# Three fp32r products for the hash bits of a bucketed attention, and another place for the chain behind them

## The reference, cut to what matters

```python
# q, k, v: (2, 8, 768, 64); proj: (64, 6)
q_bits = (einsum('bhsd,dk->bhsk', q, proj) > 0)
k_bits = (einsum('bhsd,dk->bhsk', k, proj) > 0)
q_bucket, k_bucket = sum(q_bits * 2**arange(6)), sum(k_bits * 2**arange(6))
mask   = q_bucket[:, :, :, None] == k_bucket[:, :, None, :]
scores = where(mask, q @ k.T / 8, -1e9)
attn   = exp(scores - scores.max(-1));  attn /= attn.sum(-1) + 1e-9
x      = attn @ v                       # 16 heads, 768 tokens each
x = moe(x)                              # 512 -> 2048 -> 512, leaky relu
x = moe2(x)                             # 512 -> 2048 -> 512, rational function
```

## Time and profile before

| | us |
|---|---|
| profiled execution | 849.61 |
| its span, first to last instruction | 847.6 |
| TensorE busy in it | 816.2 |
| VectorE busy | 575.8 |
| ScalarE busy | 426.7 |
| GpSimd busy | 283.7 |
| end of the first head (L571) | 50.30 |
| end of the thirteenth head | 252.47 |
| end of the last head | 293.75 |

### The profile page before, as it was taken

One profiled execution on the slowest core, in us unless ns is written; L12 is line 12 of the kernel. 1 busy time (PEld: TensorE's weight loads), 2 busy tenths in 40 slices (PEclk: granted clock), 3 DMA queues, 4 the chain that ended last, 5 costly groups with the idle time before them and its releaser, 6 DMA issues.

```text
span 847.6 us, 11624 instructions
## 1 busy us (share of the span) xinstructions
PE 816.2 (96%) x3740; PEld 651.6 (77%) x3740; DVE 575.8 (68%) x886; ACT 426.7 (50%) x639; POOL 283.7 (33%) x365
## 2 busy tenths in 40 slices
PE   8899999999999799999999999998999999999996
PEld 5577777877778678888888888886788788887884
DVE  5578778787887455445333544359998788879885
ACT  1577768777777711112011210136676666667663
POOL 5366655636545499600000044555600000000000
PEclk9999999999999999999999999999999999999999
DMA  6465664575555243200000012122100100010001
GB/s 161 122 191 150 153 157 128 149 173 142 143 131 122 70 144 121 78 1 1 0 1 1 1 50 75 54 72 74 50 2 0 50 0 0 0 49 2 0 1 49
DMA packets 33988, 60.77 MB, mean 72 GB/s; under 512 B 10016, under 2 KB 12192, under 8 KB 33952
## 3 DMA queue, kind: packets, MB, share of 16 engines
q1 hardware_dynamic: 33952, 60.30, 25.9%
HBM read 29.51 MB, written 3.19 MB: 39 GB/s over the span
## 4 chain that ended last, share of the span: by engine, by line
PE 55%; DVE 6%; ACT 2%; issue 2%; DMA 1%; DVEq 0%; ACTq 0%
PE ps_h L980 28%; PE acc L998 27%; DVE work L1137 1%; DVE num L1141 1%; DVE num L1125 1%; DMA out<-stage 1%; DVE g_lo L1102 1%; DVE work L1131 1%; ACT work L1055 1%; DVE den_q L1118 1%; ACT work L1052 1%; DVE num L1121 0%; DVE x_lo L1150 0%; ACT g_hi L1032 0%; ACT work L1041 0%
## 5 line engine op out<-in xcount | busy, mean ns | idle before, releaser
L1032 ACT ACTIVATE g_hi<-num 128x512 fp32r<-128x512 f32 x96 | 60.9, 634 | 219.2 <-PE acc L998 200.7
L1108 DVE TENSOR_SCALAR num<-ps_h,alpha_sb 128x512 f32<-128x512 f32 x48 | 36.0, 751 | 135.7 <-PE ps_h L980 135.7
L754 DVE TENSOR_REDUCE row_max<-ps_a 128x1 f32<-128x384 f32 x192 | 97.9, 552 | 23.4 <-PE ps_a L411 22.5
L551 ACT ACTIVATE ps_s<-ps_s 128x768 f32<-128x768 f32 x96 | 76.7, 798 | 52.5 <-PE ps_s L446 52.0
L782 DVE TENSOR_TENSOR p_lo<-ps_s,p_hi 128x768 fp32r<-128x768 f32 x96 | 90.8, 946 | 16.6 <-ACT p_hi L555 16.6
L555 ACT ACTIVATE p_hi<-ps_s 128x768 fp32r<-128x768 f32 x96 | 78.0, 812 | 4.6
L1102 DVE TENSOR_TENSOR g_lo<-num,g_hi 128x512 fp32r<-128x512 f32 x96 | 73.6, 767 | 8.1 <-ACT g_hi L1032 1.4
L980 PE MATMUL ps_h<-x_hi,w_late_in_hi 128*128 128x512 f32 (+1 forms) x288 | 79.0, 396 | 0.0
L980 PE MATMUL ps_h<-x_hi,w_late_in_lo 128*128 128x512 f32 (+1 forms) x288 | 78.8, 396 | 0.0
L980 PE MATMUL ps_h<-x_lo,w_late_in_hi 128*128 128x512 f32 (+1 forms) x288 | 78.8, 395 | 0.0
L1040 ACT ACTIVATE den_q<-ps_h,abs_b 128x512 f32<-128x512 f32 x48 | 33.1, 690 | 84.8 <-PE ps_h L980 69.9
(11 more groups left out here) (127 smaller groups left out, 1760.8 us busy)
## 6 DMA issues: line engine op xcount, KB each, us to landing
stage<-in_w_in SPq DMA_DIRECT2D x26, 256.0 KB, 2.8
stage<-in_w_out SPq DMA_DIRECT2D x26, 256.0 KB, 3.1
raw<-in_qk SPq DMA_DIRECT2D x16, 384.0 KB, 3.1
q<-hi SPq DMA_DIRECT2D x32, 192.0 KB
k<-hi SPq DMA_DIRECT2D x32, 192.0 KB
v_raw<-in_v SPq DMA_DIRECT2D x16, 192.0 KB, 3.0
qa<-hi SPq DMA_DIRECT2D x16, 192.0 KB
ka<-hi SPq DMA_DIRECT2D x16, 192.0 KB
```

Source lines behind the costliest of these rows:

```text
L551: nc.scalar.activation(p32, p32, ACT.Exp, scale=float(D) ** -0.5).then_inc(s_exp, 1)
L754: dve.tensor_reduce(row_max[slot][:, i, c:c + 1], ps_a[:, i, 0:HALF], AX.X, ALU.max).then_inc(s_a_free, 1)
L1032: nc.scalar.activation(g_hi[f % 2][:], num[f % 4][:], ACT.Copy).then_inc(s_ghi, 1)
L1108: dve.tensor_scalar(num[f % 4][:], h, 0.0, alpha_sb[:, f:f + 1], ALU.min, ALU.mult).then_inc(s_step, 1)
```

## The change

The bits of heads 4 to 15 no longer come from `raw` in fp32 but from `hi` and `lo` and a projection split in the same way: `pj_hi hi + pj_lo hi + pj_hi lo`, six fp32r products (kind `"split"`) in place of two fp32 ones. Heads 0 to 3 keep the fp32 products. Since `lo` is needed, the product stands behind the value products of chunk 4 and no longer in chunk 1; two `"a"` products take other places. Around it the lists of the other engines are reordered:

- ScalarE makes `hi` in chunk 3 behind `stat_rows` (before: chunk 4), `v_hi` in chunk 4 (before: chunk 1).
- GpSimd makes `lo`, then `pen`, then `v_lo`. Before, `v_lo` came first, then `pen`, then `lo`.
- SyncE's `fill_a` is cut in two. `fill_a_rows` stands right behind `load_raw`; `fill_a_bits` stands behind `store_rows`, `spread` and `load_v`, and ahead of `fill_b`. `load_raw` no longer waits for the bits product in the loop.
- The counts of finished products are taken from a table that the schedule fills, in place of formulas.

```diff
                 return [([("a", 1, 4)], [("a", 1, 5)]),
-                        ([], [("bits", 3, 0)] if bits else []),
+                        ([], [("a", 2, 0)] if more else []),
                         ([], [("m", 1, 0)]),
-                        ([], [("a", 2, 0)] if more else []),
-                        ([("a", 2, 1)] if more else [], [("a", 2, 2)] if more else []),
+                        ([], [("a", 2, 1)] if more else []),
+                        ([("a", 2, 2)] if more else [], [("split", 3, 0)] if bits else []),
                         ([], [("a", 2, 3)] if more else [])]
...
                         if left > 1:
                             load_raw(u, j + 2)
-                        if left:
-                            load_v(u, j + 1)
+                        if left > 1 or (left == 1 and u == 0):
+                            fill_a_rows(1 - u, j + 1 + u)
...
                             store_rows(sp, j - 1)
                             spread(sp, j - 1)
+                        if left:
+                            load_v(u, j + 1)
                         if left > 1 or (left == 1 and u == 0):
-                            fill_a(1 - u, j + 1 + u)
+                            fill_a_bits(1 - u, j + 1 + u)
                         if left:
                             fill_b(u, j + 1)
...
+                    elif kind == "split":
+                        pe.wait_ge(s_pjlo, 1)
+                        pe.wait_ge(s_lo, 2 * jj + slot + 1)
...
+                        elif kind == "split":
+                            pe.matmul(ps_a[:, i, 0:HALF], pj_hi[:], hi[slot][:, half], start=True, stop=False)
+                            pe.matmul(ps_a[:, i, 0:HALF], pj_lo[:], hi[slot][:, half], start=False, stop=False)
+                            m = pe.matmul(ps_a[:, i, 0:HALF], pj_hi[:], lo[slot][:, half], start=False, stop=True)
...
+                nc.scalar.activation(pj_hi[:, 0:4 * BITS], pj[:], ACT.Copy).then_inc(s_pjhi, 1)
...
-                            if c == 4 and (left > 1 or (left == 1 and u == 0)):
-                                split_qk(1 - u, j + 1 + u)
-                            if c == 1 and not (final and u == 1):
+                            if c == 4 and not (final and u == 1):
                                 split_v(1 - u, j + u)
                             if c == 3 and not (final and u == 1):
                                 stat_rows(1 - u, j + u)
+                            if c == 3 and (left > 1 or (left == 1 and u == 0)):
+                                split_qk(1 - u, j + 1 + u)
...
                             row_stats(1 - u, h + 1)
-                            split_v(1 - u, h + 1)
...
                         if left > 1 or (left == 1 and u == 0):
+                            split_qk(1 - u, j + 1 + u)
+                        if left > 1 or (left == 1 and u == 0):
                             bit_rows(1 - u, j + 1 + u)
-                            split_qk(1 - u, j + 1 + u)
+                        if not (final and u == 1):
+                            split_v(1 - u, h + 1)
...
+                dve.wait_ge(s_pjhi, 1)
+                dve.tensor_tensor(pj_lo[:, 0:4 * BITS], pj[:], pj_hi[:, 0:4 * BITS], ALU.subtract).then_inc(s_pjlo, 1)
```

More of the change, by code:

```diff
@@ L136, in build_program @@
             pj = sb("pj", [P, 4 * BITS])
+            pj_hi = sb("pj_hi", [P, P], F32R)
+            pj_lo = sb("pj_lo", [P, P], F32R)
             raw = [sb(f"raw{u}", [P, S]) for u in range(2)]
@@ L174, in build_program @@
             s_pj0 = sem("s_pj0")
+            s_pjclear = sem("s_pjclear")
+            s_pjhi = sem("s_pjhi")
+            s_pjlo = sem("s_pjlo")
             s_id = sem("s_id")
@@ L247, in build_program, with use_counts, uses_done, halves_before @@
                     [("m", 0, 0), ("a", 1, 0), ("a", 1, 1)]
+            def use_counts():
+                done, pair_start, n = {}, [], 0
+                for kind, g, c in FIRST:
+                    n += 2
+                    done[kind, g, c] = n
+                for h in range(HEADS):
+                    if h % 2 == 0:
+                        pair_start.append(n)
+                    left = min(2, PAIRS - 1 - h // 2)
+                    for before, after in uses_of(left, h % 2, h == 0):
+                        for kind, g, c in before + after:
+                            n += 2
+                            done["bits" if kind == "split" else kind, h + g, c] = n
+                return done, pair_start
+            DONE, PAIR_START = use_counts()
+            MIDDLE = HEADS // 2
+            def uses_done(kind, g, c):
+                if isinstance(g, int):
+                    return DONE[kind, g, c]
+                return 2 * USES * g + (DONE[kind, MIDDLE, c] - 2 * USES * MIDDLE)
             def a_chunks_done(g):
-                return 2 * (KC + 2) if isinstance(g, int) and g == 0 else 2 * USES * g + 2 * (FIRST_USES - USES + 2)
+                return uses_done("a", g, KC - 1)
             def bits_done(g):
-                if isinstance(g, int) and g < 4:
-                    return 2 * (1, 2, FIRST_USES + 2, FIRST_USES + 4)[g]
-                return 2 * USES * g + 2 * (FIRST_USES - 3 * USES + 3)
+                return uses_done("bits", g, 0)
             def turned(g):
[L262 to L271, removed]
+                return uses_done("m", g, 0)
+            def halves_before(j):
+                if isinstance(j, int):
+                    return PAIR_START[j]
+                return 4 * USES * j + (PAIR_START[2] - 8 * USES)
             def over_pairs(eng, body):
@@ L299, in fill_a, with fill_a_rows @@
                 def fill_a(u, jj):
+                    fill_a_rows(u, jj)
+                    fill_a_bits(u, jj)
+                def fill_a_rows(u, jj):
                     g = 2 * jj + u
@@ L306, in fill_a, with fill_a_bits @@
                     sp.dma_start(ka[u][0:D].bitcast(F32), hi[u][D:P].bitcast(F32)).then_inc(s_a_in[u], 16)
+                def fill_a_bits(u, jj):
+                    g = 2 * jj + u
                     sp.wait_ge(s_pen, g + 1)
@@ L330, in load_raw @@
                     sp.wait_ge(s_lo, g - 1)
-                    if isinstance(g, int):
+                    if isinstance(g, int) and g < 6:
                         sp.wait_ge(s_a_out, bits_done(g - 2))
-                    else:
-                        sp.wait_ge(s_a_out, 2 * USES * g - (12 * USES - bits_done(4)))
                     sp.dma_start(raw[u][:], qk[bass.ds(g, 1)].rearrange("a p s -> (a p) s")).then_inc(s_raw[u], 16)
@@ L400, in use @@
                         pe.wait_ge(s_raw[slot], 16 * (jj + 1))
-                    elif c == 0:
+                    elif kind == "a" and c == 0:
                         pe.wait_ge(s_a_in[slot], 64 * (jj + 1))
+                    elif kind == "split":
+                        pe.wait_ge(s_pjlo, 1)
+                        pe.wait_ge(s_lo, 2 * jj + slot + 1)
                     for i in range(2):
@@ L497, in pair @@
                     final = not left
-                    n = halves_before(j, left)
+                    n = halves_before(j)
                     for u in range(2):
@@ L583, in _ @@
                 split_qk(0, 1)
+                act.wait_ge(s_pj, 32)
+                act.wait_ge(s_pjclear, 1)
+                nc.scalar.activation(pj_hi[:, 0:4 * BITS], pj[:], ACT.Copy).then_inc(s_pjhi, 1)
                 def pair(j, left):
@@ L690, in _ @@
                 last.then_inc(s_clear, 1)
+                nc.gpsimd.memset(pj_hi[:].bitcast(F32), 0.0)
+                nc.gpsimd.memset(pj_lo[:].bitcast(F32), 0.0).then_inc(s_pjclear, 1)
                 pool.wait_ge(s_cst, 16)
@@ L748, in use @@
                     g = 2 * jj + slot
-                    if kind == "bits" and due(g):
+                    if kind != "a" and due(g):
                         dve.wait_ge(s_pen, g)
```

## The result

The changed kernel takes 861.45 us (median of 4 runs, 860.2 to 863.41) against 849.74 for the kernel before beside it (849.24 to 850.51): ratio 1.0141, 95% interval 1.0129 to 1.0153. It is slower by 11.7 us, where 7.6 were forecast. The profiled execution took 861.34; that of the kernel before took 849.61.

A forecast was written before the change was run, and what follows sets the result against it. The copies' landing, second limit behind TensorE (96% busy), was to set the pace through a loop. Losses of 7.5 (heads 2 to 12) and 1.0 (head 13), gain 0.9 (head 1): 7.6 onto 849.61, 857.2 us, range 852 to 861.

The forecast's parts named there:

- a loop through `fill_a_bits` and `fill_b`: SyncE's `fill_b` stands behind `fill_a_bits`, waiting for `pen`; once a head, 17.34 us (odd) or 17.66 (even) against 16.84.
- first copy to last landing: From the first of `fill_b`'s eight copies to the landing of the last: 7.96 us, bounds about 7.4 and 8.4.
- to the product: From the last landing, `stat_rows` to the end of chunk 4's value products: 4.13 us.
- product to the next `fill_b`: From the late bits product through sign bits, `pen` and two small copies to the next `fill_b`: 5.25 us.
- The product saves 0.3: Six fp32r products take 1.08 us instead of 1.40 for two fp32 ones: 0.3 saved in each of 12 heads.
- The guard instruction shortens: VectorE's guard instruction on `den` in even heads falls from 1.05 to 0.17 us once GpSimd's `pen` is elsewhere.
- The spread's cover: In even heads SyncE's `store_rows` and `spread` are done at 15.2, `pen` ready at 15.94: covered by some 0.7 us.
- `v_lo`: GpSimd's `v_lo`, now behind `pen`, is ready 4.5 us after the product's start; value products start at 4.6: hidden by 0.1.
- The setup: The once-only rounded projection on ScalarE and VectorE falls into idle time: costs nothing, at most 1 us lost.
- The sum over heads 2 to 12: Six even heads at 17.66 and five odd at 17.34: 192.7 us against 185.2, a loss of 7.5.
- copies not late: Rival: `fill_b` still starts at the head's end, so 12 heads gain 0.9 each: 838.8 us; chance 0.06.
- the tensor engine decides: Rival: TensorE bounds the attention too, so each of 12 products saves 0.3, 3.6 in all: 846.0 us; chance 0.12.

The follow-up runs named there:

- experiment 3: Changed kernel with the bits of heads 4 to 15 in the new place from `raw` in fp32 (two products, not six): 867.16 us, ratio 1.0197.
- experiment 1: Changed kernel with ScalarE, not SyncE, issuing the two `fill_a_bits` copies behind its evacuation: 849.32 us, ratio 0.9996.
- experiment 2: Kernel before, with two small spare copies issued ahead of `fill_b` in heads 3 to 15: 868.42 us, ratio 1.0224.
- experiment 6: Changed kernel with the even heads' reciprocals of the denominators in chunk 3 instead of chunk 2: 866.92 us, ratio 1.0195.
- experiment 7: Six of `fill_b`'s eight copies issued once the score products are through: on experiment 5 (new order) 843.11 us; alone on the kernel before (old order) 849.0 us.
- experiment 4: Changed kernel with 12 small filler products ahead of chunk 3's `a` product: heads 1 to 13, 862.46 us; heads 2 to 11 only, 861.73 us.
- experiment 5: Kernel of experiment 1 with the load of v moved back behind `load_raw`, ahead of `fill_b`: 846.76 us, ratio 0.9968.
- experiment 8: Kernel of experiment 7's new order with GpSimd's weight splits moved behind head 1's row statistics and to head 14: 838.68 us, ratio 0.9871.

## Why the prediction was right, and where it was off

The forecast, slower by a loop through `fill_a_bits` and `fill_b`, was right in place and in mechanism, and 857.2 was 4.3 low. The terms below are nearly all right; the miss is what the sum had no term for. The signs named for it came: `fill_b` 1.50 to 1.59 after the evacuation in the steady heads, over 1 us of waiting for `k<-pen` in heads 2 to 13, and a guard instruction of 0.17.

| term | forecast | measured |
|---|---|---|
| first copy to last landing | 7.96 | 8.02 (194.76 to 202.78) |
| to the product | 4.13 | 4.05 (to 206.83) |
| product to the next `fill_b` | 5.25 | 5.29 (to 212.12) |
| odd head | 17.34 | 17.36; periods 17.43 to 17.46 |
| issue of `den`, its landing | 6.22 + 2.18 | 6.25 + 2.18 (176.98, 183.23, 185.41) |
| guard instruction to `p_lo` | 0.35 | 0.35 (to 185.76) |
| `p_lo` to the product | 3.66 | 3.59 (to 189.35) |
| product to the next `fill_b` | 5.25 | 5.41 (to 194.76) |
| even head | 17.66 | 17.78; periods 17.47 to 17.69 |
| head 13, loss | 1.0 | 1.35 |
| head 1, gain | 0.9 | 0.71 |

- *The product saves 0.3.* Right, 0.3 to 0.35 in experiment 3, in undisturbed heads.
- *The move holds `fill_b`.* Shown from both sides: experiment 1 takes the wait off SyncE's queue and the loss goes; experiment 2 makes `fill_b` late with nothing else and loses more.
- *The guard instruction shortens.* Right: 0.17 with `pen` elsewhere. With `pen` beside it 1.11 in experiment 2, with `lo` beside it 1.23 in experiment 6, and 0.94 in experiment 7's old order. The Trainium skill, "SBUF — State Buffer", section "Who interferes with whom", has tensor_scalar among the VectorE operations that can contend with GpSimd for the shared port pair, and says that the engine which issued second fully blocks. These rows agree: each time the GpSimd instruction had started first, and the guard instruction ended within 0.04 us of it. The prediction gave the rule without that condition on the operation.
- *The spread's cover, `v_lo`, the setup.* The cover held in the steady heads. It did not in head 2's list: `pen` ended at 84.13 and `fill_a_bits` started at 84.63, behind `store_rows` (1.31 to issue), the spread and the load of v, which is the 0.4 of head 3. No wait for `v_lo` shows. The setup cost 0.4 at most (head 0).
- *What was mis-sized.* The sum over heads 2 to 12: 7.5 forecast, 12.7 measured. 7.6 of it is the loop; 5.1 lies in heads 3, 6 and 10, at 1.2 GHz for some 3.4 us each (0.4 of head 3 apart, as said). I had no term for TensorE's clock, although the sum itself made VectorE, and so TensorE, stand still for `den` or `k<-pen` in every head. The 2.2 that the feed-forward start gave back wasn't in it either. Added up for the profiled executions: 7.6 + 1.35 (head 13) - 0.7 (head 1) + 0.4 (head 0) - 0.1 (head 14) + 5.1 - 2.2 = 11.4, the difference of the spans. That the clock cost 4.7 of it rests on the rows of these heads; experiment 4 did not bring it back in the median.
- *The rival "copies not late", 838.8.* Its condition could be met, but its price was wrong: it took 7.96 as fixed. Two queues issuing at once stretch it, and it took three more moves (experiments 5, 7 and 8) to come to 838.7. That this is so near 838.8 is chance: experiments 7 and 8 remove waits that the rival's sum doesn't hold.
- *The rival "the tensor engine decides".* In no head from 1 to 14 of the changed kernel, where `stat_rows` waits for `k<-pen` throughout; in experiment 7's new order TensorE releases it. How much of the 5.9 us there is the product's saving and how much the new order's is not separated.

## What to carry to other kernels

A DMA queue that issues in order passes every wait on to what stands behind it: before a step is moved, look at which copies are queued behind its issue, and whether they close a loop from one iteration to the next. Here the loop was priced to a tenth of a microsecond a head from rows of the old trace; what a sum of this kind misses is the clock, so where it predicts new idle time of TensorE, a term or a wider upper end belongs in it. And work that nobody waits for, like the split of weights here, must not stand ahead of a short chain that the next step needs.

## What of the hardware was not expected

- In the kernel after the granted clock fell to 0.50 (1.2 GHz) for about 3.4 us in three of the heads 2 to 12: in head 10 behind idle times of 1.11 and 0.46 us, in head 6 behind 1.11 and 0.49, in head 3 behind 1.66. Nearly the same idle times in the head from 175.48 (1.12 and 0.46) had no such effect. What picks the heads is open.
- A small VectorE instruction of 0.17 us took 0.94 to 1.23 beside a GpSimd instruction and ended with it, for two different GpSimd instructions.
- While ScalarE issued copies at the same time, SyncE's fourth copy took 0.89 to 1.29 us to issue and the eight landed after 8.5 to 8.7 (experiment 5, heads 3 to 12). In head 14 of the same kernel, where ScalarE issues none, it was 0.60 and 7.96. With the load of v just ahead of the eight the landing took 9.0 to 9.2 (experiment 1, odd heads from 5).
- The same small `den` copy landed in 2.17 or in 3.60 us in the same place of two kernels that differ in TensorE's work alone (kernel after and experiment 4).
